# An empty first pass for the expert loop on TensorE, surplus groups inside it, seven one-hot rows on ScalarE

## The reference

```python
# 1: gated linear attention, 4 x 8 heads, 768 steps, head_dim 48
state = f[:, :, t, :, None] * state + einsum('bhd,bhe->bhde', k[:, :, t], v[:, :, t])
y[:, :, t] = einsum('bhd,bhde->bhe', q[:, :, t], state)
# 2: mixture of 8 experts, one expert per token, hidden size 1024
expert_idx = argmax(xn @ en.T / tau, axis=1)
out[mask] = gate_w[mask, None] * (maximum(x[mask] @ w1[e], 0.0) @ w2[e])
# 3: gated feed-forward, hidden size 1536
return ((x @ w_a) * (x @ w_b)) @ w_out
```

## Time and profile before

| | us |
|---|---|
| median of 3 runs | 831.78 (829.67 to 832.59) |
| profiled execution | 830.27, of it 829.0 in the span of the profile |
| PE busy | 810.1 (98%), 5400 matmuls |
| PE weight loads | 736.9 |
| DVE, ACT, POOL busy | 364.4, 321.6, 141.1 |

### The profile page before, as it was taken

One profiled execution on the slowest core, in us unless ns is written; L12 is line 12 of the kernel. 1 busy time (PEld: TensorE's weight loads), 2 busy tenths in 40 slices (PEclk: granted clock), 3 DMA queues, 4 the chain that ended last, 5 costly groups with the idle time before them and its releaser, 6 DMA issues.

```text
span 829.0 us, 14425 instructions
## 1 busy us (share of the span) xinstructions
PE 810.1 (98%) x5400; PEld 736.9 (89%) x5401; DVE 364.4 (44%) x597; ACT 321.6 (39%) x608; POOL 141.1 (17%) x206
## 2 busy tenths in 40 slices
PE   5999998989999999999999999999999999999998
PEld 4999987989999999998888888888888888888887
DVE  6788877836453645356532322232232223222221
ACT  5677775435453545355421321231222212212211
POOL 4544440423232322100000100010010001001001
PEclk9999999999999999999999999999999999999999
DMA  9777752556552554320000100010010001000001
GB/s 211 194 207 193 201 176 88 110 192 212 206 174 92 207 199 155 125 77 1 0 1 1 39 1 0 1 39 1 0 39 1 1 1 38 1 1 10 28 1 39
DMA packets 32572, 67.57 MB, mean 82 GB/s; under 512 B 12145, under 2 KB 21390, under 8 KB 31374
## 3 DMA queue, kind: packets, MB, share of 16 engines
q1 hardware_dynamic: 28174, 55.93, 22.0%
q0 software_dynamic: 4352, 11.04, 4.3%
HBM read 57.48 MB, written 9.48 MB: 81 GB/s over the span
## 4 chain that ended last, share of the span: by engine, by line
PE 97%; DVE 1%; issue 1%; DMA 0%; ACT 0%; POOL 0%; DVEq 0%
PE low_banks L1024 18%; PE scores L1024 18%; PE sums L1031 9%; PE high_banks L1031 9%; PE sums L978 8%; PE low_banks L967 6%; PE scores L967 6%; PE high_banks L978 4%; PE scores L812 3%; PE sums L828 3%; PE high_banks L801 2%; PE sums L819 2%; PE low_banks L787 2%; PE low_banks L795 1%; PE high_banks L839 1%; PE sums L901 1%
## 5 line engine op out<-in xcount | busy, mean ns | idle before, releaser
L568 POOL DMA_INDIRECT out<-out_sb,placed x24 | 23.3, 970 | 469.3 <-ACT out_sb L758 463.4
L1024 PE MATMUL low_banks<-x_hi,wab_lo 128*128 128x512 f32 x216 | 84.7, 392 | 0.0
L1024 PE MATMUL scores<-x_hi,wab_lo 128*128 128x512 f32 x216 | 84.7, 392 | 0.0
L1024 PE MATMUL low_banks<-yT_lo,wab_hi 128*128 128x512 f32 x216 | 84.6, 392 | 0.0
L1024 PE MATMUL scores<-yT_lo,wab_hi 128*128 128x512 f32 x216 | 84.6, 392 | 0.0
L1024 PE MATMUL low_banks<-x_hi,wab_hi 128*128 128x512 f32 x216 | 84.0, 389 | 0.0
L1024 PE MATMUL scores<-x_hi,wab_hi 128*128 128x512 f32 x216 | 84.0, 389 | 0.0
L1417 DVE TENSOR_TENSOR h<-low_banks,a_sb 128x512 f32<-128x512 f32 x36 | 25.0, 693 | 132.4 <-ACT a_sb L741 132.4
L1417 DVE TENSOR_TENSOR h<-scores,a_sb 128x512 f32<-128x512 f32 x36 | 25.0, 693 | 130.2 <-ACT a_sb L741 117.9
L741 ACT ACTIVATE a_sb<-low_banks 128x512 f32<-128x512 f32 x36 | 21.6, 599 | 137.8 <-PE low_banks L1024 137.8
L741 ACT ACTIVATE a_sb<-scores 128x512 f32<-128x512 f32 x36 | 21.6, 599 | 134.5 <-PE scores L1024 134.5
(11 more groups left out here) (229 smaller groups left out, 1867.8 us busy)
## 6 DMA issues: line engine op xcount, KB each, us to landing
w_raw<-in_w SPq DMA_DIRECT2D x8, 1536.0 KB
w_raw<-in_w SPq DMA_DIRECT2D x32, 384.0 KB
tok<-in_tok SPq DMA_DIRECT2D x48, 192.0 KB, 3.2
qk_all<-in_chan SPq DMA_DIRECT2D x48, 192.0 KB, 3.3
xd<-xst SPq DMA_DIRECT2D x24, 192.0 KB, 1.9
wab_raw<-in_wab SPq DMA_DIRECT2D x6, 768.0 KB, 6.6
wout_raw<-in_wout SPq DMA_DIRECT2D x1, 1536.0 KB, 6.4
wout_raw<-in_wout SPq DMA_DIRECT2D x1, 768.0 KB, 4.3
```

The source lines that it names most:

```text
L568: pool.indirect_dma_start(out=out, out_offset=bass.IndirectOffsetOnAxis(ap=placed[:, u * B + t, 0:1].bitcast(i32), axis=0), in_=out_sb[:, ...
L1024: last_op = pe.matmul(bank[2 * i + m][:, :], w[:, KM * m + k, cols], moving, start=(k == 0 and w is wab_hi and x is not None), stop=(k == ...
```

## The change

PE enters the expert loop directly behind the rank product, and the loop has nine passes. In pass 0 it skips both copies of the group and the surplus code, runs the inversion, the transposes of three tiles of group 0 and, if group 0 is wide, of its fourth tile. Passes 1 to 8 each run one group (`i * 7 // 8` is i - 1 for them). Inside a group the fourth tile of the next group is transposed only if that group is wide; if not, one small matmul counts the semaphore in its place. Surplus groups, if any, run inside pass 8 behind group 7. The 13 warm-up matmuls behind the rank product are gone. DVE makes 17 of the one-hot rows; ACT makes the other seven as relu(1 - (low - column)^2): seven `Square` into the new tile `off` and one `Relu`. SP's `w2` loads wait for the first one-hot row, and POOL waits for its last gather into the fourth tile before it starts the next one.

```diff
+    BY_DVE = 17
+    off = sb("off", [P, TILES - BY_DVE, P], f16)
@@ SP
         sp_eng.wait_ge(ssq_ready, TILES)
+        sp_eng.wait_ge(low_ready, 1)
         for i in range(PAIRS):
             load_w2(slice(0, P), i)
@@ POOL, gather_x
                 if j:
                     pool.wait_ge(x1T_done, j * TB - TB + t + 1)
+                    if t == TB - 1:
+                        pool.wait_ge(xin_loaded[t], j * 16)
@@ ACT
         act.activation(r["norm"][:, :], ssq_all[:, :], ACT.Sqrt).then_inc(norm_ready, 1)
+        act.wait_ge(low_known, 1)
+        for i in range(BY_DVE, TILES):
+            act.activation(off[:, i - BY_DVE, :], column[:, :], ACT.Square, bias=r["low"][:, i:i + 1], scale=-1.0).then_inc(rest_ready, 1)
+        act.wait_ge(rest_ready, TILES - BY_DVE)
+        act.activation(in_low[:, BY_DVE:, :], off[:, :, :], ACT.Relu, bias=1.0, scale=-1.0).then_inc(rest_ready, 1)
@@ PE
-        keep_warm(13)
-        (inversion, keep_warm(15), transpose_x with its fill: now the functions invert() and transpose_tile(j, t))
+        def transpose_fourth(j, wide):
+            with pe.If(wide > 0):
+                transpose_tile(j, TB - 1)
+            with pe.If(wide < 1):
+                pe.matmul(bank[TB - 1][0:32, 0:E], every[:, 0:32], every[:, 0:E], start=True, stop=True).then_inc(x1T_done, 1)
@@ PE, group
             up(j, n)
+            if i is not None:
+                wide = pe.value_load(tile_wide[0:1, bass.ds(i, 1)], min_val=0, max_val=1)
             pe.wait_ge(y_copied, j * KM + 1)
             down(j, 0, n, True)
-            with pe.If(i < FULL - 1):
-                transpose_x(j + 1)
+            if i is not None:
+                with pe.If(i < FULL):
+                    for t in range(TB - 1):
+                        transpose_tile(j + 1, t)
+                    transpose_fourth(j + 1, wide)
@@ PE, loop
-        transpose_x(0, fill=3)
-        pe.wait_ge(groups_ready, 1)
-        more = ...; with pe.If(more > 0): surplus loop
-        with pe.Fori(0, FULL) as i: ...
+        with pe.Fori(0, FULL + 1) as i:
+            with pe.If(i > 0):
+                j = i * (FULL - 1) // FULL
+                chosen = pe.value_load(tile_wide[0:1, bass.ds(j, 1)], min_val=0, max_val=1)
+                pe.wait_ge(x1l, j * TB + TB)
+                with pe.If(chosen < 1):
+                    group(j, 3 * P, i)
+                with pe.If(chosen > 0):
+                    group(j, TW, i)
+            with pe.If(i > FULL - 1):
+                more = pe.value_load(tiles_used[0:1, 2:3], min_val=0, max_val=NT - FULL)
+                with pe.If(more > 0):
+                    (the surplus groups, with their own transposes)
+            with pe.If(i < 1):
+                invert()
+                for t in range(TB - 1):
+                    transpose_tile(0, t)
+                    keep_warm(3)
+                pe.wait_ge(groups_ready, 1)
+                wide = pe.value_load(tile_wide[0:1, 0:1], min_val=0, max_val=1)
+                transpose_fourth(0, wide)
@@ DVE
-        link(dve.tensor_copy(r["low"][:, :], place_low[:, :]))
+        dve.tensor_copy(r["low"][:, :], place_low[:, :]).then_inc(low_known, 1)
+        dve.wait_ge(low_known, 1)
-        for i in range(TILES):
+        for i in range(BY_DVE):
             dve.tensor_scalar(in_low[:, i, :], ...)
```

More of the change, by code:

```diff
@@ L265, in attention_moe_ffn @@
         sem, ("norm_ready", "ex_ready", "diff_ready", "prefix_ready", "rank_done"))
+    low_known, rest_ready = map(sem, ("low_known", "rest_ready"))
     low_ready, inverted, token_ready, tokenT_done, table_ready, table_stored = map(
@@ L937, in _, with invert, transpose_tile @@
         pe.matmul(bank[0][:, E:2 * E + 1], every[:, :], r["pre"][:, 0:E * TILES + 1:TILES], start=True, stop=True).then_inc(rank_done, 1)
-        keep_warm(13)
-        for i in range(TILES):
[L941 to L956, removed]
+        def invert():
+            for i in range(TILES):
+                if i < BY_DVE:
+                    pe.wait_ge(low_ready, i + 1)
+                else:
+                    pe.wait_ge(rest_ready, TILES - BY_DVE + 1)
+                last_op = pe.matmul(bank[1][:, 0:TILES], in_low[:, i, :], in_block[:, i, :],
+                                    start=(i == 0), stop=(i == TILES - 1))
+            last_op.then_inc(inverted, 1)
+            pe.wait_ge(token_ready, 2)
+            pe.wait_ge(x_ready, TILES + 1)
+            pe.transpose(bank[6][0:TILES, 0:P], r["token"][:, :], ident[:, :]).then_inc(tokenT_done, 1)
+            keep_warm(15)
+        def transpose_tile(j, t):
+            pe.wait_ge(xin_loaded[t], j * 16 + 16)
+            for k in range(KM):
+                last_op = pe.transpose(bank[t][:, P * k:P * k + P], xin[:, t, P * k:P * k + P], ident[:, :])
+            last_op.then_inc(x1T_done, 1)
+        def transpose_fourth(j, wide):
[3 more added lines that the diff above has]
+                pe.matmul(bank[TB - 1][0:32, 0:E], every[:, 0:32], every[:, 0:E], start=True, stop=True).then_inc(x1T_done, 1)
         def up(j, n):
@@ L988, in group @@
             for m in range(1, KM):
                 down(j, m, n, False)
-        transpose_x(0, fill=3)
-        pe.wait_ge(groups_ready, 1)
[L993 to L1006, removed]
+        with pe.Fori(0, FULL + 1) as i:
[10 more added lines that the diff above has]
+                with pe.If(more > 0):
+                    with pe.Fori(0, NT - FULL) as extra:
+                        with pe.If(extra < more):
+                            for t in range(TB):
+                                transpose_tile(extra + FULL, t)
+                            pe.wait_ge(x1l, extra * TB + FULL * TB + TB)
+                            group(extra + FULL, TW, None)
+            with pe.If(i < 1):
[6 more added lines that the diff above has]
+                transpose_fourth(0, wide)
```

## The result

The changed kernel takes 839.87 us (median, 839.43 to 840.95) against 831.56 for the kernel before: a ratio of 1.0104, 95% interval 1.0084 to 1.0125. It is slower by 8.3 us; the forecast was 827.9 with a range up to 832.5. The profiled span is 837.9 us, 8.9 more than before.

The account below looks back on a forecast made before the run. PE was taken as the bound, busy 98% of the span. Terms -2.90 - 1.0 - 0.4 + 0.4 = -3.9 from the profiled 830.27 gave 826.4, or 827.9 as a median; range 826.0 to 832.5.

Parts of the forecast that it names:

- What bounds the kernel: Whole kernel: PE busy 98% of the span; the 2.90 us gap at 181.78 is code that had to be fetched.
- The end of the first group: End of group 0: code behind both copies, reached in pass 0, is there, so the gap goes, -2.90 us.
- third rival: PE's loop: only an unbroken run of blocks is kept; way back +4.1, group 0's end +8.9, about 842; chance 0.13.
- What the empty pass costs: Pass 0: two jumps past unfetched code delay the inversion's end, +0.4 us, between -0.8 and +2.2, or +4.
- fourth rival: PE's loop: only the present block and the next are kept; eight ways back pay 2.90 or more, some 851; chance 0.02.
- The one-hot rows: Before the inversion: seven fewer rows on DVE end 1.16 us sooner; without a new obstacle the inversion ends 0.8 us sooner.
- The fourth tile: Narrow groups: one small matmul replaces three transposes, -1.0 us for four groups; group 0's path shortens by 0.4 us.
- The sequencer's time in hand: Between groups: of 1.6 us in hand, added branches and register steps take some 0.5, so 1.1 us stay.

Follow-up runs that it names:

- e1: Kernel before with 56 dead instructions added inside the surplus loop, which never runs here; 827.26 us, ratio 0.9956.
- e3: Changed kernel with one more empty pass in front, so two empty passes; 844.2 us in one run.
- e4: Kernel before with only the one-hot rows split 17 to 7 between VectorE and ScalarE; 830.89 us, ratio 0.9999.
- e7: e1 plus the fourth tile's transposes only where the next group is wide, else one small matmul; 827.1 us, ratio 0.9956.
- e2: Changed kernel with the condition i > 0 written around each group copy separately, each with its own width load; 835.46 us, ratio 1.0061.

## Why the prediction was wrong, point by point

**What bounds the kernel**: right. The gap of 2.90 us was a fetch, as read from the earlier trace rows, and e1 removed it without touching an executed instruction.

**The end of the first group**: the step that failed. It said that code reached in pass 0 is there when group 0 ends, and priced this at -2.90 us. It was +6.5 us in the gap and +2.6 us of lower clock behind it. The first only the third rival had, the second no case. The conclusion from the earlier trace rows that all code of the loop stays was taken from a loop whose blocks had all been fetched in order. The prediction saw that no row showed a jump over a whole block, and wrote it down under the third rival, but gave the unseen case 0.13 and the term one value. It bounded the cost of the empty pass from both sides; done here in the same way, with the three branches of its third rival, the term would have reached from -2.9 to +6.0, and the range with it.

**The third rival** named the place and the three slow branches (2.90 and 3.0 twice, in the trace a gap of 9.42 in all) and gave 842 against 839.9. Its sum has an error: the 8.9 us are the whole new gap, of which the kernel before already has 2.90, so the added time is 6.0, and its terms make +9.1 (839.4 for a profiled run, measured 839.65), not +12.0. Its mechanism was half right: the way back from pass 0 took 0.22 us, not 4.48, so blocks ahead of the gap stay, and by e3 those beyond it stay too until the skipped block is fetched. The 4.1 us for the way back that didn't come were made up by the 2.6 us of clock that it had left out, 0.5 us more in the gap and 0.8 us of savings that were not there. That the sum comes so near is luck.

**The fourth rival** (two blocks) fell: nine ways back in 0.08 to 0.23 us. The Trainium skill (Runtime: NRT & Kernel Launch, section Instruction fetch mechanics) has both: a memory refilled like a queue, which fits what e3 shows, and a window of two pages, which the rows contradict.

**What the empty pass costs**: two waits of 3.90 and 2.99 us, taken as 4.48 or 2.95 and 3.0. The code was there at 143.6, inside the predicted 143.1 to 143.8. The 24 products took 0.81 us at the lower clock (granted 0.50), not 1.4. So the inversion ended at 144.57, +0.05 us instead of +0.4.

**The one-hot rows**: DVE's last was ready at 143.22 (said: 143.1), as timed; but PE's code came at 143.6, so the 0.8 us were spent on the empty pass. Alone (e4) they gave nothing that the runs can tell.

**The fourth tile**: said -1.0 and -0.4 us, measured -0.2 for four groups by the timeline and nothing that the runs of e7 can tell; the small matmul stands behind the branches, not 0.03 us behind its neighbour. In group 0 it stands behind the third tile's warm-up matmuls, at 153.41, so it came when the fourth tile used to.

**The sequencer's time in hand**: right for the change (no new gap in later groups), and e2 shows that a second load of the width in each pass breaks it.

## What to carry to other kernels

Before an idle stretch with no semaphore behind it is attacked, look at the sequencer's branches and at the engine's instruction queue: every branch of 3 us or more was a fetch here, and its price depended on where the code happened to lie. Shift the code by some dozens of dead instructions first (8 did nothing here, 56 closed the gap); it is the cheapest test, and no other edit here gave more. A dry pass warmed the loop only where every block of it was fetched in that pass (e2); here the blocks beyond a skipped one had to be fetched again after the skipped one had come.

## What the runs showed of the hardware

- PE's program came in packets of 16 KB. A branch to a block not yet asked for took 3.9 to 5.2 us of the sequencer, one to a block just asked for 3.0 to 3.5 and once 4.2 (e3, pass 0, the row below); taken to a present block it was 0.20 to 0.25 (0.44 once, in e2 at 136.2), and not taken 0.07 to 0.08.

```profile
L1032 PEldq COMPARE_BRANCH  x1: 4172/4172/4172, 143.7 to 143.7; - x1
```

- The blocks of the nine-pass loop stayed once they had been fetched in order, with no packet from 192 to 386 us. They are seven by the packets, with the one behind the loop: 123.6, 130.8, 165.2 (the skipped one), 179.8, 183.0, 186.6 and 189.8 us.
- Blocks beyond a skipped one were usable over a way back (0.22 and 0.21 us in e3), and were fetched again after the skipped one had come (4.38 and 3.31 us). Why is not shown.
- After 9.42 us without a matmul PE ran 18 matmuls at the lower clock, at a cost of 2.6 us. It varies: in e3, after 9.54 us, only nine ran at it (granted 0.50 from 197.21 to 200.00), and the first 18 took 4.80 us, 1.4 more than the 3.40 before. After the 2.90 us of the kernel before the clock was at its upper level.
- Left open: whether the changed loop with a stepping stone but without the second load of the width would be worth anything. It wasn't tried. An estimate from the traces: e2's first group at 156.99 and the 218.97 us that e1 takes from there to the feed-forward (155.37 to 374.34) give 376.0, against 377.34 before and 374.34 in e1. So it may gain something, but less than the dead code.
